# Two transforms and two expert layers on one core: first products moved ahead in TensorE's order, a second place for v, and GpSimd's first operations tied to VectorE's

## What is computed

```python
def _attn_ref(x):                       # x: (2, 3008, 256)
    X = np.fft.fft(x, axis=1)
    X = np.fft.fft(X, axis=2)
    return X.real.astype(np.float32)

def _moe_ref(x, w_in, w_out):           # 6016 tokens, 256 -> 2048 -> 256
    h = x @ w_in
    g = h * (1.0 / (1.0 + np.exp(-h)))
    return (g @ w_out).astype(np.float32)

def _moe2_ref(x, w_in, w_out, alpha):
    h = x @ w_in
    g = np.maximum(h, 0.0) + alpha * np.minimum(h, 0.0)
    return (g @ w_out).astype(np.float32)

# reference: moe2(moe(attn(x)))
```

## Time and profile before

| | before |
|---|---|
| median of 3 runs | 934.2 us (933.95 to 934.76) |
| the profiled execution, its own time | 933.09 us |
| its span in the profile | 931.2 us |
| granted TensorE clock | 0.999 of full speed |
| TensorE matmul busy | 923.3 us, 99% |
| VectorE busy | 635.2 us, 68% |
| GpSimd busy | 594.4 us, 64% |
| ScalarE busy | 551.6 us, 59% |

### The profile page before, as it was taken

How to read it: one execution, slowest core, us unless ns; L and a number is a source line. 1 busy time by engine, 2 the same in 40 slices (tenths; PEclk the granted TensorE clock), 3 DMA queues, 4 the chain that set the end, 5 groups by cost and what they waited for, 6 DMA issues and landing times.

```text
span 931.2 us, 11837 instructions
## 1 busy us (share of the span) xinstructions
PE 923.3 (99%) x4034; PEld 757.2 (81%) x4034; DVE 635.2 (68%) x967; ACT 551.6 (59%) x858; POOL 594.4 (64%) x408
## 2 busy tenths in 40 slices
PE   9999999999999999999999999999999999999998
PEld 4588887788888888888888888888888888888886
DVE  6879996455545545544877777777777777778774
ACT  4575654567667656676665565465555555555544
POOL 0496555259959859676697476566747756664443
PEclk9999999999999999999999999999999999999999
DMA  9512100020020120100300200020020002001001
GB/s 361 222 56 68 45 1 1 1 67 23 13 78 23 55 80 1 45 1 1 124 11 1 71 20 1 0 89 1 1 88 1 1 1 89 1 1 44 1 1 45
DMA packets 19826, 40.35 MB, mean 43 GB/s; under 512 B 1803, under 2 KB 15669, under 8 KB 18741
## 3 DMA queue, kind: packets, MB, share of 16 engines
q1 hardware_dynamic: 18980, 39.05, 11.9%
q10 hardware_dynamic: 688, 0.52, 0.2%
q0 software_dynamic: 96, 0.02, 0.0%
HBM read 27.22 MB, written 12.37 MB: 43 GB/s over the span
## 4 chain that ended last, share of the span: by engine, by line
PE 94%; DVE 2%; POOL 1%; DMA 1%; ACT 1%; issue 0%; SPq 0%; DVEq 0%; ACTq 0%; POOLq 0%
PE ps L354 12%; PE ps L352 12%; PE ps L353 12%; PE ps L668 9%; PE ps L671 9%; PE ps L667 9%; PE ps L613 9%; PE ps L609 9%; PE ps L610 9%; DMA x_tile<-x_tiles 1%; PE ps L556 1%; POOL gl L1313 1%; PE ps L541 1%; PE ps L537 1%; POOL wo L1248 0%
## 5 line engine op out<-in xcount | busy, mean ns | idle before, releaser
L1335 POOL TENSOR_TENSOR gl<-g,gh 128x502 fp32r<-128x502 f32 x192 | 224.8, 1178 | 175.3 <-ACT gh L857 175.3
L1313 POOL TENSOR_TENSOR gl<-g_sb,gh 128x1004 fp32r<-128x1004 f32 x96 | 210.3, 2190 | 121.2 <-ACT g_sb L814 119.2
L851 ACT ACTIVATE g<-ps 128x502 f32<-128x502 f32 x192 | 111.9, 591 | 110.3 <-DVE ps L1196 105.3
L1148 DVE SCALAR_TENSOR_TENSOR h_sb<-n_all,a,v_sb 128x502 f32<-128x502 f32 x96 | 83.1, 865 | 135.1 <-ACT v_sb L876 135.0
L1203 DVE SCALAR_TENSOR_TENSOR g<-g,less_alpha,ps 128x502 f32<-128x502 f32 x192 | 132.6, 732 | 31.9 <-ACT g L851 31.8
L609 PE MATMUL ps<-gh,wo 128*128 128x502 f32 x384 | 148.8, 388 | 0.3
L610 PE MATMUL ps<-gh,wo 128*128 128x502 f32 x384 | 147.9, 385 | 0.0
L667 PE MATMUL ps<-gh,wo 128*128 128x502 f32 x382 | 147.3, 386 | 0.0
L668 PE MATMUL ps<-gh,wo 128*128 128x502 f32 x382 | 147.3, 386 | 0.0
L857 ACT CAST gh<-g 128x502 fp32r<-128x502 f32 x192 | 113.0, 614 | 40.3 <-DVE g L1203 38.6
L876 ACT COPY v_sb<-ps 128x502 f32<-128x502 f32 x96 | 55.6, 580 | 122.5 <-PE ps L354 118.4
(11 more groups left out here) (132 smaller groups left out, 1618.4 us busy)
## 6 DMA issues: line engine op xcount, KB each, us to landing
x_tile<-x_tiles SPq DMA_DIRECT2D x6, 1024.0 KB, 13.5
x_rows<-x SPq DMA_DIRECT2D x6, 1004.0 KB, 5.9
out_t<-out_sb SPq DMA_DIRECT2D x11, 502.0 KB, 3.2
x_raw_b<-x_rows SPq DMA_DIRECT2D x18, 251.0 KB, 4.0
stage<-moe_w_out SPq DMA_DIRECT2D x16, 256.0 KB, 4.5
n_parts<-n_rows SPq DMA_DIRECT2D x5, 502.0 KB, 3.7
stage<-moe_w_in SPq DMA_DIRECT2D x8, 256.0 KB, 5.0
w_sb<-moe_w_in SPq DMA_DIRECT2D x3, 512.0 KB, 7.8
```

Source lines behind the costliest of these rows:

```text
L851: act.activation(g4[:, k, :], product_bank(u, TILE_IN[k]), ACT.Relu, scale=-1.0).then_inc(relu_done, 1)
L1313: pool.tensor_tensor(gl[g % 2][:, :, :], g_sb[g % 2][:, :, :], gh[g % 2][:, :, :].bitcast(F32), ALU.subtract).then_inc(gl_done, 1)
L1335: pool.tensor_tensor(gl4[:, k, :], g4[:, k, :], gh4[:, k, :].bitcast(F32), ALU.subtract).then_inc(gl_done, 1)
```

## The change

1. TensorE: `first1(1)` comes directly behind `first1(0)`, with its wait for `n_done`, and `transform23(3, 0, "q")` behind it.
2. v of step g=1 goes to half of `n_parts`, a tile that is first loaded later; so ScalarE's copy waits for `h_done` from g=2 on only.
3. VectorE: `ab_low(4)` and `ab_low(5)` come ahead of the first step instead of behind it.
4. GpSimd: `split_lo(0)` waits for `w_done` of step 0 and comes ahead of `ab_low(7)`, which waits for `w_done` of step 1.

```diff
--- before.py
+++ after.py
@@ -112,6 +112,7 @@
         mt = at("mt", OPA_AT, [P, 2, FEATW], F32)
         w_sb = at("w_sb", OPA_AT + 2048, [P, 2, FF], F32)
         n_all0 = at("n_all0", OPA_AT, [P, N], F32)
+
         v_sb = at("v_sb", OPA_AT + 2016, [P, N], F32)
         h_sb = [at(f"h_sb{i}", OPA_AT + (4032, 12288)[i], [P, 2, N], F32) for i in range(2)]
         n_parts = at("n_parts", OPA_AT + 8192, [P, 2, N], F32)
@@ -369,6 +370,10 @@
         def half_last(n):
 
             return STEPS1 + 4 * HF * (n + 1)
+
+        def v_of(g):
+
+            return n_parts[:, 0, :] if g == 1 else v_sb[:, :]
 
         block = ctx.enter_context(nc.Block())
 
@@ -703,10 +708,10 @@
             transform23(3, 0, "p")
             spread_n0()
             first1(0)
+            pe.wait_ge(n_done, 1)
+            first1(1)
             pe.wait_ge(a2_done, 1)
             transform23(3, 0, "q")
-            pe.wait_ge(n_done, 1)
-            first1(1)
             job(JOB_AFTER[LAG - 1])
             for g in range(LAG, STEPS1):
                 first1(g)
@@ -871,9 +876,9 @@
 
             for g in range(STEPS1):
                 act.wait_ge(mm1, g + 1)
-                if g >= 1:
+                if g >= 2:
                     act.wait_ge(h_done, g)
-                act.copy(v_sb[:, :], pair(g)[:, 1, :]).then_inc(v_done, 1)
+                act.copy(v_of(g), pair(g)[:, 1, :]).then_inc(v_done, 1)
                 if g == 0:
                     split_hi(1)
                 if g >= 1:
@@ -1132,6 +1137,8 @@
             t23_low(2, 0, "q")
             t1_late_low(0, "p")
             t1_late_low(0, "q")
+            ab_low(4)
+            ab_low(5)
 
             def store_x1_plus(c):
                 dve.wait_ge(mm2, NF * (c + 1))
@@ -1146,9 +1153,9 @@
                     dve.wait_ge(n_done, g // NF + 1)
                     dve.wait_ge(a2_done, 1)
                 dve.scalar_tensor_tensor(out=h[:, 1, :], in0=n_all[g // NF % 2][:, :],
-                                         scalar=a2[:, g % NF:g % NF + 1], in1=v_sb[:, :],
+                                         scalar=a2[:, g % NF:g % NF + 1], in1=v_of(g),
                                          op0=ALU.mult, op1=ALU.subtract).then_inc(w_done, 1)
-                dve.tensor_tensor(h[:, 0, :], pair(g)[:, 0, :], v_sb[:, :], ALU.add)
+                dve.tensor_tensor(h[:, 0, :], pair(g)[:, 0, :], v_of(g), ALU.add)
                 dve.wait_ge(w_done, g + 1)
                 dve.tensor_tensor(h[:, 1, :], pair(g)[:, 0, :], h[:, 1, :], ALU.add).then_inc(h_done, 1)
                 if g % NF == LAG - 1 and g >= NF:
@@ -1170,9 +1177,6 @@
                     t1_late_low(1, former[2])
                 elif former == "t3":
                     n_hold_low()
-                if g == 0:
-                    ab_low(4)
-                    ab_low(5)
                 if g in FOLD_AFTER:
                     i = FOLD_AFTER.index(g)
                     fold_piece(QT + i // 7, i % 7)
@@ -1303,10 +1307,13 @@
             pool.wait_ge(ab_lo, 2)
             ab_low(2)
             ab_low(3)
+
             pool.wait_ge(t1_lo, 2)
             ab_low(6)
+            pool.wait_ge(w_done, 1)
+            split_lo(0)
+            pool.wait_ge(w_done, 2)
             ab_low(7)
-            split_lo(0)
             for g in range(STEPS1):
                 pool.wait_ge(gh_done, g + 1)
                 pool.wait_ge(silu_done, g + 1)
```

## The result

The changed kernel takes 932.6 us in the median of 17 runs, against 934.2 for the kernel before in 17 runs; the ratio is 0.9984, with a 95% interval of 0.9976 to 0.9992. That is 1.5 us (0.7 to 2.2) or 0.16% less. The interval excludes a ratio of 1, and the gain lies inside the 0.2% that the prediction set as what a measurement tells from no change. Forecast were 932.8 and the same band.

A forecast was written before the change was run, and what follows sets the result against it. GpSimd, without a break from gl(1), sets when the products on gl(7) start; TensorE alone bounds what follows. -0.90 (lock, less moved ab_low) and -0.48 (v(1) off the path) make -1.38, so 934.2 becomes 932.8; range 931.6 to 934.5.

The forecast's parts named there:

- the same band: Whole kernel: time within 0.2% (1.87 us) of before, about what can't be told from no change; chance 0.69.
- The lock between VectorE and GpSimd: VectorE operations with two SBUF inputs and GpSimd ones reading SBUF block each other; first scalar_tensor_tensor 0.73, not 1.70.
- -0.90 for h of g=0: VectorE's first step: lock avoided at L1087 and the first scalar_tensor_tensor, less moved ab_low; h done at 38.24, not 39.14.
- -0.48 for v(1): ScalarE: v(1) no longer waits for h of g=0, so silu(0) starts 0.09 after h, at 38.33; 0.48 gained.
- What was hidden: Delays costing nothing: second scalar_tensor_tensor 0.26 late beside split_lo(0), ab_low(7) at 39.1 to 40.4, weight load at 38.5.
- rival 3: SP's weight load for split_hi(4), issued 1 us later and wanted 1.9 sooner, makes it slower by over 1.87; chance 0.04.
- -1.38 passed on to gl(1) and gl(7): Silu(0)'s gain reaches GpSimd's gl(1), 45.75 for 47.13, and the products on gl(7), 73.47, in full.
- The rounds of 4.33 stay: GpSimd's stage from gl(3) on: rounds stay 4.34, so 0 gained there, bounds 0.4 either way.
- Rival 1: GpSimd's stage shrinks too, if a fold or scalar_tensor_tensor falls into idle GpSimd: -1.7 to -3.0; chance 0.17.
- A step that was off: TensorE: first1(2) at 40.5, then 0.222 per matmul, reaching the products on gl(1) at 47.7, gl(1) ending at 47.9.
- 1.7 in reserve: TensorE's own gain at first1(2), 40.5 against 42.23, showing in the time only if GpSimd's stage shrinks.

The follow-up runs named there:

- two halves: Kernel before with only TensorE's order and v's place changed: 934.10 us; with only VectorE's ab_low ahead and GpSimd's waits: 933.74, against 933.93.
- ab_low_back: Changed kernel with VectorE's ab_low(4) and ab_low(5) behind step 0 again: ratio 0.9988 to the kernel before.
- run of late folds: Changed kernel with batch 1's folds on VectorE starting behind step 8 instead of 4, two behind some steps: ratio 1.0041 to the kernel before.
- kernel before with late folds: Kernel before with batch 1's folds on VectorE starting behind step 8 instead of 4, two behind some steps: ratio 1.0078 to the kernel before.

## Why the prediction was right

- **The lock between VectorE and GpSimd** was read rightly, down to who waits for whom. The Trainium skill, SBUF — State Buffer, "Who interferes with whom", calls the ports that the two share an exclusive lock, where the order of issue decides who blocks; the run without the waits agrees and shows it taken in turns, 1.68 and 1.71 for 1.28 on one side, 2.39 for 1.28 on the other.
- **-0.90 for h of g=0.** Measured -0.89: its last operation ends at 37.82+0.67, which is 38.25 with the 0.24 taken off, for 38.24. So the links before it: ab_low from 35.14 (35.13), the scalar_tensor_tensor from 36.34 (36.33).
- **-0.48 for v(1).** Measured -0.51, from the run with the one place for v put back; silu(0) at 38.28 (0.24 off), predicted 38.33.
- **What was hidden.** split_lo(0) makes the second scalar_tensor_tensor 0.06 longer, not 0.26, though their rows overlap by the 0.26 (38.41 to 38.67); ab_low(7) at 39.04 (predicted 39.1) and gl(0) at 40.39 (40.43), both 0.24 off. The weight load is issued at 38.5 (0.24 off), as predicted, and the four land in 2.5 to 2.8: rival 3's place has no part in the result.
- **-1.38 passed on to gl(1) and gl(7).** Measured -1.43 and -1.41. The rounds of 4.33 stay, as said. Rival 1 asked for idle time on GpSimd and there was none; with the splits spread, GpSimd got it, and the further 1.2 was there.
- **A step that was off.** first1(2) starts at 40.32 (0.24 off), 0.2 ahead of the forecast, but TensorE was to reach the products on gl(1) at 47.7, by 0.222 per matmul. It came at 48.08 (0.24 off), 0.2 after gl(1) had ended, because the 31 matmuls from 41.09 on had the pitch of 0.233, 0.3 us more in all. It cost nothing, since GpSimd was the bound behind it. The prediction gave TensorE 1.7 in reserve; it was nearer 1.4.

The time by itself would not decide: the interval of the ratio (0.7 to 2.2 us) also takes in the lower end of rival 1 (1.7). It is the profile that shows the mechanism, link by link, and the runs without single links that show each one needed. One result is no test of the chances.

## What to carry to other kernels

VectorE operations with two SBUF inputs and GpSimd operations that read SBUF make one queue; count them as a sum, put GpSimd's next operation where VectorE reads PSUM, and if it must be held back, one semaphore wait is enough. Edits on one chain of waits need not be worth the sum of their single values: here two halves gave 0 and 0.3 and together 1.4, so try them together before dropping one. And before shortening one engine's wait, ask which engine is the bound behind it: here it was GpSimd's rounds, and spreading its splits gave another 1.0 to 1.2 by the profiles.

## What the runs showed of the hardware that had not been expected

TensorE has a second pitch for these matmuls of 502 columns, 0.233 us in place of 0.223 (steps of 4.20 for 4.02), at a granted clock of 1.00 in the profile. At the start of this kernel it came where the last idle time between the transforms and the steps was gone, and an idle time of 0.27 at that place kept it away in both kernels that were given one. Going on from a transform without a gap is not enough by itself: behind the first transform of the earlier trace rows, from 37.59 on, the matmuls start 0.225 to 0.229 apart and not 0.233. Nor is the start the only place: `ab_low_back`, with 0.62 of idle time ahead of first1(2) and the pitch of 0.223 behind it, has 0.233 in its profile from about 450 us to the end, with no idle time of TensorE over 0.05 in between. What sets it off, and why it ended where it did, stays open.

In the run of late folds, a wait of TensorE of 2.0 us was followed by a granted clock of 0.50 of full speed, the 1.2 GHz level, from 113.0 to 116.4 us, in which matmuls start 0.42 apart; then it was back at 0.99. The kernel before with late folds shows the same behind its wait of 2.20.
